# Gate logits of a routed result from VectorE instead of TensorE, with GpSimd's index copies moved ahead

## The chip, the core and the metric

The program runs on one core of a Trainium2 chip. The metric is the device time of one execution in microseconds (us). Five engines run side by side: TensorE (PE in the profile, its weight loads PEld), VectorE (DVE), ScalarE (ACT), GpSimd (POOL) and SyncE (SP), which issues transfers. Engines wait for each other on semaphores. Transfers run on 16 DMA engines. PSUM is the memory that TensorE writes to, in banks of 512 fp32 numbers per partition; SBUF is the working memory.

## What is computed

A chunked attention gives 2304 rows of 512 numbers. Then come two mixtures of 8 experts. Each row goes to the expert with its largest gate logit, through two products with a ReLU between, and comes back scaled by a gate:

```
logits = x @ w_gate                       # 512 -> 8
e_idx = argmax(logits); gate_w = softmax(logits)[e_idx]
h = maximum(x[mask] @ w1[e], 0)           # 512 -> 1024
ye = h @ w2[e]                            # 1024 -> 512
out[mask] = gate_w * eom * ye             # mixture 1, eom a sigmoid of a second gate
out[i] = gate_w[i] * y[expert, pos]       # mixture 2, with a capacity of 576 rows per expert
```

The second mixture needs `logits = x @ moe2_w_gate` of the first mixture's result before it can route.

## The kernel before

In the attention (18 blocks of 128 rows) the first mixture's logits are made too, and the first 16 pieces of expert weights are loaded. Then both mixtures (m = 0 and 1) sort their rows by expert into tiles of 128, 20 tiles in each here, and go through them one a step.

Products are in fp32 precision by parts: each operand is split into a rounded high part and a low remainder, and three matmuls (high by high, low by high, high by low) make one product (`product`, L988 to L990). An expert's weights are 8 pieces of 128x1024: SyncE loads a piece into a ring of 4, ScalarE rounds it (`wh`), GpSimd subtracts (`wl`, L427). Two experts are held at a time. A piece of expert e may overwrite expert e-2 once the last tile of that one is through.

Step g on each engine, in program order:

- TensorE: transposes of the hidden rows of tile g (L1010); the first product of tile g+1 (24 matmuls), in which, in mixture 1, the four transposes of result g-1 (L1029) and its logit matmuls (L1035) are set; the transposes of the gathered rows of tile g+2 (L983); the second product of tile g (24 matmuls), into one PSUM bank.
- VectorE: splits the hidden rows into high and low (L809, L815), in mixture 1 copies the transposed result (L823) and its 8 logits (L834), ReLU of tile g+1 (L792), splits the gathered rows of tile g+2 (L800, L802), scales result g into `y` (L830) once the scatter of result g-1 has landed.
- GpSimd: loads three bounds that say how many pieces are due (`due`, L435 to L440); makes the low parts of up to 4 pieces (`split`); scatters result g-1 (`scatter`: index copy L526, transfer L532); gathers the rows of tile g+3 (`gather`: index copy L515, transfer L518), which needs TensorE's row transposes of tile g+2 done; makes the low parts of up to 4 more pieces.

A table computed from the routing sets the pieces of each step, so an expert's weights are ready about when its first tile is. `y`, the gathered rows `xg` and both index columns (`sidx`, `gidx`) have one buffer each. The queue of every engine is in order: what waits holds all that is behind it.

Of the kernel before, what the change touches and what calls it, by code (L numbers as in the profile page):

```python
# [6 lines left out]
BF16 = mybir.dt.bfloat16  # L7
# [6 lines left out]
P = 128  # L14
# [9 lines left out]
def build(nc, q, k, v, wg1, wog1, w1a, w2a, wg2, w1b, w2b, cap, out):  # L24
# [29 lines left out]
    with ctx:  # L54
# [32 lines left out]
        wgate2 = sb("wgate2", [P, DC, E])  # L87
# [57 lines left out]
        at_pos = sb("at_pos", [P, 2, P, NH2], BF16)  # L145
        in_tile = sb("in_tile", [P, 2, NTAB, NH2], BF16)
        at_tile = sb("at_tile", [P, 2, NV, NTAB, NH2], BF16)
        at_gate = sb("at_gate", [P, 2, NG, NTAB, NH2], BF16)
        xg = sb("xg", [P, ROW])
        yT = sb("yT", [P, DC, P])  # L150
        h = sb("h", [P, F])
# [12 lines left out]
        hTh = sb("hTh", [P, FC, P], F32R)  # L164
        hTl = sb("hTl", [P, FC, P], F32R)
# [13 lines left out]
        ps_h, ps_hT, ps_y, ps_yT, ps_xT = b01, b23, b45[:, 0:BANK], b45[:, BANK:2 * BANK], b6  # L179
# [5 lines left out]
        s_w = sem("s_w")  # L185
        s_zero = sem("s_zero")
# [60 lines left out]
        yT_done = sem("yT_done")  # L247
        yT_here = sem("yT_here")
        yl_done = sem("yl_done")
        yl_here = sem("yl_here")  # L250
# [6 lines left out]
        def at(x, g):  # L257

            return x[:, g:g + 1] if isinstance(g, int) else x[:, bass.ds(g, 1)]

# [44 lines left out]
        def _(sp):  # L305
# [3 lines left out]
            sp.dma_start(wgate2[:, :, :], wg2.rearrange("(c p) e -> p c e", p=P)).then_inc(s_w, 16)  # L309
# [89 lines left out]
        def _(pool):  # L399
# [56 lines left out]
            for m in range(2):  # L456
# [79 lines left out]
                def step(g, ahead=True):  # L536
# [8 lines left out]
                    split(middle, hi)  # L545

                step(0)
                with pool.Fori(1, total - 2) as g:
                    step(g)
                step(total - 2, ahead=False)  # L550
                step(total - 1, ahead=False)
                scatter(total - 1)
# [5 lines left out]
        def _(act):  # L558
# [49 lines left out]

            exponentials(0)
# [16 lines left out]
        def _(dve):  # L626
            dve.wait_ge(s_const, 2)
            dve.wait_ge(s_w, 64)
# [60 lines left out]
            for m in range(2):  # L689
# [92 lines left out]
                def gates_copy():  # L782
                    dve.wait_ge(gates_done, m + 1)
                    link(nc.vector.tensor_reduce(gates[m][:, :], ps_gate[:, 0:NG * NTAB].rearrange("p (a c) -> p c a", a=NG),
                                                 AX.X, ALU.add))

# [32 lines left out]
                def y_copy(j):  # L819
                    dve.wait_ge(yT_done, j + 1)  # L820
                    if reached(j, 1):
                        dve.wait_ge(yl_done, j)
                    nc.vector.tensor_copy(yT[:, :, :], ps_yT.rearrange("p (c t) -> p c t", c=DC)).then_inc(yT_here, 1)  # L823

                def scaled(j):
# [4 lines left out]
                    nc.vector.tensor_scalar(y[:, 0:D], ps_y, at(gates[m], j), None, ALU.mult).then_inc(y_here[m], 1)  # L830

                def logits_copy(j):
                    dve.wait_ge(yl_done, j + 1)
                    nc.vector.tensor_copy(y[:, D:ROW], ps_yT[:, 0:E]).then_inc(yl_here, 1)  # L834

                def step(g, head=False, tail=False):
                    if head:
                        dve.wait_ge(routed, m + 1)
                        x_split(0)
# [8 lines left out]
                    if m == 0 and reached(g, 1):  # L848
                        y_copy(g - 1)
# [3 lines left out]
                    if m == 0 and reached(g, 1):  # L853
                        logits_copy(g - 1)
# [11 lines left out]
        def _(pe):  # L866
            pe.wait_ge(s_const, 2)
            pe.wait_ge(s_w, 64)
# [71 lines left out]
            for m in range(2):  # L940
# [72 lines left out]
                def second_product(g, first, before):  # L1013
                    pe.wait_ge(wl_here, before + PX)
                    if reached(g, 1):
                        pe.wait_ge(y_here[m], g)
                    for half in range(2):
                        pe.wait_ge((hT0_here, hT1_here)[half][m], g + 1)
                        for c in range(half * FC // 2, (half + 1) * FC // 2):
                            last = product(ps_y, hTh[:, c, :], hTl[:, c, :], (first, D * F // P // BANK + c),  # L1020
                                           start=(c == 0), stop=(c == FC - 1))
                    last.then_inc(y_done[m], 1)

                def result_T(j):
                    pe.wait_ge(y_here[m], j + 1)
                    if reached(j, 1):
                        pe.wait_ge(yl_here, j)
                    for c in range(DC):
                        last = nc.tensor.transpose(ps_yT[:, c * P:(c + 1) * P], y[:, c * P:(c + 1) * P], ident[:, :])  # L1029
                    last.then_inc(yT_done, 1)  # L1030

                def result_logits(j):
                    pe.wait_ge(yT_here, j + 1)
                    for c in range(DC):
# [57 lines left out]
```

## Time and profile before

| | |
|---|---|
| median of 3 runs | 767.88 us (763.83, 767.88, 769.28) |
| profiled execution | 763.25 us, span 761.4 us, mean granted TensorE clock 0.934 of full |
| busy share of the span | PE 86%, PEld 71%, POOL 55%, DVE 45%, ACT 22% |
| first mixture | steps from 145 us, last scatter 436.83 us |
| second mixture | steps from 480 us, last scatter 751.99 us |
| chain that ended last | PE 63%, POOL 10%, issue 9%, DVE 6%, DMA 5% |

The span is the time from the first to the last instruction. A busy share is an average over stages: attention up to 117 us, routing to 134 us, first mixture to 440 us, routing to 468 us, second mixture to the end.

### The profile page before, as it was taken

The page shows a single profiled execution, that of the slowest core. Times are in us where ns is not written, and L with a number is a line of the kernel's source. Part 1 is how long each engine was busy: PE and PEld are TensorE (multiplying, and loading weights), DVE is VectorE, ACT ScalarE, POOL GpSimd, SP SyncE. Part 2 cuts the span into 40 slices and gives each one's busy share as a digit, 9 for nine tenths or more (in the row PEclk, how much of TensorE's full clock was granted, in tenths as well). Part 3 has the DMA queues.
Part 4 walks back from the last instruction along what each step waited for, and adds up shares of the span by engine and source line. Part 5 has one row for each costly group of instructions (what it writes and reads, how often), then busy time and mean ns, then how long its engine had stood idle before and what let it go on. Part 6 is the DMA issues. An engine that isn't in the chain of part 4 may idle for free.

```text
span 761.4 us, 15861 instructions
## 1 busy us (share of the span) xinstructions
PE 654.5 (86%) x4742; PEld 540.3 (71%) x4743; DVE 344.6 (45%) x634; ACT 170.2 (22%) x205; POOL 420.5 (55%) x351
## 2 busy tenths in 40 slices
PE   4799984899999999998998623999999999999553
PEld 3698973688887888887876422788888878887442
DVE  2465657345444545434433266454545354532240
ACT  1465650002230222213224200002122210233300
POOL 1355553113786638778877524116648763679760
PEclk9999996799999999999999755999999999999796
DMA  7999988011454324454455314014225533355510
GB/s 168 277 277 269 291 261 280 28 34 60 154 207 167 110 78 165 169 191 155 170 189 173 125 15 135 29 42 151 96 92 182 167 131 111 95 183 187 190 42 22
DMA packets 79694, 111.71 MB, mean 147 GB/s; under 512 B 28249, under 2 KB 46681, under 8 KB 79664
## 3 DMA queue, kind: packets, MB, share of 16 engines
q1 hardware_dynamic: 69344, 86.05, 36.7%
q0 software_dynamic: 8000, 25.17, 9.9%
q8 instruction: 21, 0.34, 0.2%
q10 hardware_dynamic: 2320, 0.07, 0.2%
q14 instruction: 9, 0.07, 0.0%
HBM read 92.48 MB, written 20.00 MB: 148 GB/s over the span
## 4 chain that ended last, share of the span: by engine, by line
PE 63%; POOL 10%; issue 9%; DVE 6%; DMA 5%; POOLq 4%; ACT 1%; SPq 0%; ACTq 0%; DVEq 0%
PE b L988 15%; PE b L989 14%; PE b L990 14%; POOL wl L427 8%; PE b L915 5%; PE b L1010 3%; PE b L937 2%; DMA qin<-in_q 2%; PE b L983 2%; PE b L1035 2%; PE b L929 2%; PE b L892 1%; PE b L884 1%; DVE owner L761 1%; POOLq L427 1%
## 5 line engine op out<-in xcount | busy, mean ns | idle before, releaser
L427 POOL TENSOR_TENSOR wl<-ring,wh (+1 forms) x128 | 302.4, 2390 | 41.1 <-ACT wh L600 21.0
L600 ACT CAST wh<-ring 128x1024 f32 (+1 forms) x112 | 112.8, 1047 | 482.4 <-PE b L990 389.8
L988 PE MATMUL b<-wh,xTh 128*128 x320 | 134.8, 421 | 5.9 <-DVE xTl L802 3.7
L988 PE MATMUL b<-wh,hTh 128*128 x320 | 132.0, 413 | 7.5 <-DVE hTl L815 7.5
L830 DVE TENSOR_SCALAR y<-b,gates 128x512 f32<-128x512 f32 x40 | 30.0, 750 | 227.1 <-PE b L990 102.5
L989 PE MATMUL b<-wh,xTl 128*128 x320 | 128.7, 402 | 0.0
L989 PE MATMUL b<-wh,hTl 128*128 x320 | 128.6, 402 | 0.0
L990 PE MATMUL b<-wl,hTh 128*128 x320 | 127.5, 398 | 0.0
L990 PE MATMUL b<-wl,xTh 128*128 x320 | 127.5, 398 | 0.0
L792 DVE TENSOR_SCALAR h<-b 128x512 f32<-128x512 f32 x80 | 54.8, 689 | 77.9 <-PE b L990 77.7
L988 PEld LDWEIGHTS b<-wh,hTh 128*128 128x128 f32 x320 | 61.5, 192 | 21.1 <-issue 7.7
L988 PEld LDWEIGHTS b<-wh,xTh 128*128 128x128 f32 x320 | 61.3, 192 | 19.2 <-issue 7.4
L990 PEld LDWEIGHTS b<-wl,hTh 128*128 128x128 f32 x320 | 61.2, 191 | 15.0
L990 PEld LDWEIGHTS b<-wl,xTh 128*128 128x128 f32 x320 | 61.2, 191 | 14.8
L989 PEld LDWEIGHTS b<-wh,hTl 128*128 128x128 f32 x320 | 61.5, 192 | 12.7
L989 PEld LDWEIGHTS b<-wh,xTl 128*128 128x128 f32 x320 | 61.5, 192 | 11.2
L518 POOL DMA_INDIRECT xg<-x,gidx x36 | 37.9, 1052 | 31.6 <-POOL gidx L515 31.6
L815 DVE TENSOR_TENSOR hTl<-b,hTh 128x512 fp32r<-128x512 f32 x80 | 52.6, 679 | 0.0
L809 DVE CAST hTh<-b 128x512 fp32r<-128x512 f32 x80 | 51.1, 680 | 0.0
L983 PE MATMUL b<-ident,xg 128*128 128x128 f32 x168 | 26.8, 284 | 25.4 <-DMA xg<-x,gidx 12.3
L532 POOL DMA_INDIRECT x<-y,sidx x20 | 20.5, 1024 | 49.8 <-DVE y L834 26.6
L431 POOL DMA_DIRECT2D x<-xrow x18 | 10.3, 570 | 64.5 <-DVE xrow L664 64.5
(142 smaller groups left out, 667.4 us busy)
## 6 DMA issues: line engine op xcount, KB each, us to landing
ring<-in_moe_w SPq DMA_DIRECT2D x128, 512.0 KB, 3.3
vin<-in_v SPq DMA_DIRECT2D x72, 64.0 KB, 4.7
x<-xrow POOLq DMA_DIRECT2D x18, 256.0 KB, 5.9
out<-zeros SPq DMA_DIRECT2D x18, 256.0 KB, 3.2
qin<-in_q SPq DMA_DIRECT2D x6, 512.0 KB, 7.3
kin<-in_k SPq DMA_DIRECT2D x6, 512.0 KB, 7.5
qin<-in_q SPq DMA_DIRECT2D x2, 384.0 KB, 8.2
kin<-in_k SPq DMA_DIRECT2D x2, 384.0 KB, 8.3
```

The source lines that it names most:

```text
L427: nc.gpsimd.tensor_tensor(low, src, high.bitcast(F32), ALU.subtract).then_inc(wl_here, 1)
L518: nc.gpsimd.indirect_dma_start(xg[:, 0:src.shape[1]], None, src, bass.IndirectOffsetOnAxis(ap=gidx[:, 0:1], axis=0), bounds_check=N - 1, o ...
L600: nc.scalar.copy(dst, ring[:, i % RING]).then_inc(wh_here, 1)
L792: nc.vector.tensor_scalar_max(h[:, cols], ps_h[:, cols], 0.0).then_inc((h0_here, h1_here)[half][m], 1)
L809: nc.vector.tensor_copy(hTh[:, chunks, :], ps_hT[:, half * BANK:(half + 1) * BANK].rearrange("p (c t) -> p c t", t=P)).then_inc((hTh0_here ...
L815: nc.vector.tensor_tensor(hTl[:, chunks, :], ps_hT[:, half * BANK:(half + 1) * BANK].rearrange("p (c t) -> p c t", t=P), hTh[:, chunks, :] ...
L830: nc.vector.tensor_scalar(y[:, 0:D], ps_y, at(gates[m], j), None, ALU.mult).then_inc(y_here[m], 1)
L915: last = nc.tensor.matmul(b01[e * DH:(e + 1) * DH, u * BANK + g * P:u * BANK + (g + 1) * P], src[:, n // 2 % QS, g, e, u, :], ident[:, :], ...
L983: last = nc.tensor.transpose(ps_xT[:, c * P:(c + 1) * P], xg[:, c * P:(c + 1) * P], ident[:, :])
L988: nc.tensor.matmul(dst, high, weights(wh, *wt), start=start, stop=False)
L989: nc.tensor.matmul(dst, low, weights(wh, *wt), start=False, stop=False)
L990: return nc.tensor.matmul(dst, high, weights(wl, *wt), start=False, stop=stop)
```

## The change

Four edits go together.

1. The second mixture's logits no longer come from TensorE. The gate matrix is handed over transposed (8 rows of 512) and broadcast to all partitions in one transfer from ScalarE's queue (`wg2_rows`, 2 MB in SBUF). VectorE makes logit e of a result as one instruction: PSUM result times gate times row e, and the sum over 512 numbers (`scalar_tensor_tensor` with `accum_out`), eight per tile. The transposes, the copy of the transposed result and the logit matmuls go.
2. The second product alternates between two PSUM banks (`result_bank`), in both mixtures. In mixture 1 result g-1 is scaled at the end of VectorE's step g, behind the eight sums; `y_here` starts at one more, so the second product of tile g waits for the scaling of g-2.
3. In mixture 1 the scatter is two steps behind (`behind`).
4. GpSimd copies the index columns at the end of a step, for the next step's gather and scatter (`next_gather`, `next_scatter`), instead of right before each transfer.

Some SBUF tiles are laid over others to make room.

```diff
+        def result_bank(eng, j):
+            if isinstance(j, int):
+                return b45[:, j % 2 * BANK:(j % 2 + 1) * BANK]
+            return b45[:, bass.ds(eng.snap((j % 2) * BANK), BANK)]
...
+                def next_gather(g):
+                    if reached(g, 4):
+                        pool.wait_ge(g_in[m], g * 16)
+                    nc.gpsimd.tensor_copy(gidx[:, :], at(gather_at[m], g)).then_inc(gi_here[m], 1)
+
+                def next_scatter(g):
+                    if reached(g, 1):
+                        pool.wait_ge(y_out[m], g * 16)
+                    nc.gpsimd.tensor_copy(sidx[:, :], at(scatter_at[m], g)).then_inc(si_here[m], 1)
                 def gather(g):
-                    if reached(g, 1):
-                        pool.wait_ge(g_in[m], g * 16)
-                        pool.wait_ge(xT_done[m], g)
-                    nc.gpsimd.tensor_copy(gidx[:, :], at(gather_at[m], g)).then_inc(gi_here[m], 1)
+                    pool.wait_ge(xT_done[m], g)
...
                 def scatter(g):
-                    if reached(g, 1):
-                        pool.wait_ge(y_out[m], g * 16)
-                    nc.gpsimd.tensor_copy(sidx[:, :], at(scatter_at[m], g)).then_inc(si_here[m], 1)
                     pool.wait_ge(si_here[m], g + 1)
-                    pool.wait_ge(y_here[m], g + 1)
-                    if m == 0:
-                        pool.wait_ge(yl_here, g + 1)
+                    pool.wait_ge(y_here[m], g + 2)
...
                     lo, middle, hi = due(m, g)
                     split(lo, middle)
-                    if reached(g, 1):
-                        scatter(g - 1)
+                    if reached(g, behind):
+                        scatter(g - behind)
                     if ahead:
                         gather(g + 3)
                     split(middle, hi)
+                    if ahead:
+                        next_gather(g + 4)
+                    if reached(g, behind - 1):
+                        next_scatter(g + 1 - behind)
+                behind = (2, 1)[m]
...
+            act.wait_ge(lg_done, NT)
+            act.wait_ge(o_done, NT)
+            act.wait_ge(x_here, NT)
+            act.dma_start(wg2_rows[:, :, :].rearrange("p e d -> p (e d)"),
+                          wg2.rearrange("e d -> (e d)").unsqueeze(0).partition_broadcast(P)).then_inc(wg2_in, 16)
...
+                def next_logits(j, experts):
+                    dve.wait_ge(y_done[m], j + 1)
+                    dve.wait_ge(y_here[m], j + 1)
+                    for e in experts:
+                        if e >= 2:
+                            dve.wait_ge(next_lg_here, j * E + e - 1)
+                        nc.vector.scalar_tensor_tensor(
+                            out=(unread, b7)[e % 2][:, :], in0=result_bank(dve, j), scalar=at(gates[m], j), in1=wg2_rows[:, e, :],
+                            op0=ALU.mult, op1=ALU.mult, accum_out=next_lg[:, e:e + 1]).then_inc(next_lg_here, 1)
...
                     if m == 0 and reached(g, 1):
-                        logits_copy(g - 1)
+                        next_logits(g - 1, range(0, E // 2))
                     if not tail:
                         relu(g + 1, 1)
                         x_split(g + 2)
-                    scaled(g)
+                    if m == 0 and reached(g, 1):
+                        next_logits(g - 1, range(E // 2, E))
+                        scaled(g - 1)
                     if m == 0 and tail:
-                        y_copy(g)
-                        logits_copy(g)
+                        next_logits(g, range(E))
+                    if m == 1 or tail:
+                        scaled(g)
```

GpSimd's queue in the loop of the first mixture, from the first group of pieces to the next step's bounds, before (`sidx` and `gidx` are the index columns, `y_out0` and `g_in0` count landed scatters and gathers):

```order
L526 ISA [waits y_out0]
L526 COPY sidx<-scatter_at 128x1
L532 DMA x<-y,sidx 2304x520 [waits yl_here,si_here0,y_here0]
L513 ISA
L515 ISA [waits xT_done0,g_in0]
L515 COPY gidx<-gather_at 128x1
L518 DMA xg<-x,gidx 128x512 [waits gi_here0]
```

The same place now; the rows left out are the second group of pieces:

```order
L544 DMA x<-y,sidx 2304x520 [waits si_here0,y_here0]
L532 REGISTER_ALU
L535 DMA xg<-x,gidx 128x512 [waits xT_done0,gi_here0]
...
L522 ISA [waits g_in0]
L522 COPY gidx<-gather_at 128x1
L527 REGISTER_ALU
L528 ISA [waits y_out0]
L528 COPY sidx<-scatter_at 128x1
```

The copies and the waits for landed transfers have moved from in front of the transfers to the end of the step, ahead of the next step's bounds.

VectorE's queue in the same loop, second half of a step, before (`h`, `xTh`, `xTl` belong to later tiles, `y` is the scaled result):

```order
L792 TENSOR_SCALAR h<-b 128x512 [waits hT0_done0,h0_done0]
L834 COPY y<-b 128x8 [waits yl_done]
L792 TENSOR_SCALAR h<-b 128x512 [waits hT1_done0,h1_done0]
L797 REGISTER_ALU
L800 CAST xTh<-b 128x512 [waits h1_done0,xT_done0]
L802 TENSOR_TENSOR xTl<-b,xTh 128x512 [waits xTh_here0]
L829 REGISTER_ALU [waits y_done0]
L830 ISA [waits y_out0]
L830 TENSOR_SCALAR y<-b,gates 128x512
```

And the end of that step now, behind the split of the gathered rows (four sums stand ahead of the second ReLU in the same way):

```order
L832 TENSOR_TENSOR xTl<-b,xTh 128x512 [waits xTh_here0]
L866 REGISTER_ALU [waits y_here0,y_done0]
L867 SCALAR_TENSOR_TENSOR unread,next_lg<-b,gates,wg_rows 128x512 [waits next_lg_here]
L866 REGISTER_ALU
L867 SCALAR_TENSOR_TENSOR b,next_lg<-b,gates,wg_rows 128x512 [waits next_lg_here]
...
L853 REGISTER_ALU [waits y_done0]
L855 REGISTER_ALU [waits y_out0]
L856 COPY y<-next_lg 128x8 [waits next_lg_here]
```

The wait for the scatter's landing still ends VectorE's step, now behind four more 128x512 instructions and for the result of one step earlier.

## Rows read from the trace of the kernel before

**Rows 1.** Timeline of TensorE, steps of both mixtures: start us, us, engine, instruction.
```profile
173.10 1.03 PE L1010 MATMUL b<-ident,h 128*128 128x128 f32 x8
...
180.91 0.60 PE L983 MATMUL b<-ident,xg 128*128 128x128 f32 x4
...
186.94 1.03 PE L1010 MATMUL b<-ident,h 128*128 128x128 f32 x8
...
581.38 1.03 PE L1010 MATMUL b<-ident,h 128*128 128x128 f32 x8
593.89 1.03 PE L1010 MATMUL b<-ident,h 128*128 128x128 f32 x8
```

**Rows 2.** Timeline of GpSimd, one full step; in brackets idle time before, and its releaser.
```profile
284.07 9.43 POOL L427 TENSOR_TENSOR wl<-ring,wh  x4 [1.57 <-issue]
...
294.54 1.03 POOL L532 DMA_INDIRECT x<-y,sidx  x1 [0.92 <-PE b L983]
...
296.63 1.06 POOL L518 DMA_INDIRECT xg<-x,gidx  x1 [0.86 <-POOL gidx L515]
299.30 9.43 POOL L427 TENSOR_TENSOR wl<-ring,wh  x4 [1.62 <-issue]
```

**Rows 3.** Timeline of GpSimd, first mixture, steps 2 to 4 and step 9.
```profile
182.82 1.05 POOL L518 DMA_INDIRECT xg<-x,gidx  x1 [0.85 <-POOL gidx L515]
185.49 9.45 POOL L427 TENSOR_TENSOR wl<-ring,wh  x4 [1.61 <-ACT wh L600]
...
202.59 9.47 POOL L427 TENSOR_TENSOR wl<-ring,wh  x4 [3.43 <-ACT wh L600]
...
279.35 1.03 POOL L532 DMA_INDIRECT x<-y,sidx  x1 [7.77 <-DVE y L834]
```

**Rows 4.** The page's costliest groups, two of VectorE: busy, mean ns, idle before.
```profile
L830 DVE TENSOR_SCALAR y<-b,gates 128x512 f32<-128x512 f32 x40 | 30.0, 750 | 227.1 <-PE b L990 102.5
...
L815 DVE TENSOR_TENSOR hTl<-b,hTh 128x512 fp32r<-128x512 f32 x80 | 52.6, 679 | 0.0
```

**Rows 5.** Windows: length, PE, PEld, DVE, ACT, POOL busy, clock, DMA share, GB/s.
```profile
115.00:120.00 5.00, 2.02 (x15) 1.59 (x14) 2.35 (x8) 0.91 (x2) 1.09 (x2) 0.81 0.99 369
...
130.00:135.00 5.00, 3.30 (x20) 2.61 (x18) 2.70 (x16) 0.00 (x0) 1.11 (x1) 0.50 0.19 52
...
186.00:200.00 14.00, 14.00 (x74) 11.66 (x73) 6.66 (x11) 0.00 (x0) 11.36 (x8) 1.00 0.51 171
```

**Rows 6.** All 36 gathers of line L518: issue to landing.
```profile
DMA to landing us min/median/max: 3.2/3.4/4.2
```

**Rows 7.** Timeline of GpSimd, end of the first mixture.
```profile
404.99 9.47 POOL L427 TENSOR_TENSOR wl<-ring,wh  x4 [1.61 <-ACT wh L600]
...
415.50 1.03 POOL L532 DMA_INDIRECT x<-y,sidx  x1 [0.92 <-POOL sidx L526]
...
428.56 1.02 POOL L532 DMA_INDIRECT x<-y,sidx  x1 [0.94 <-POOL sidx L526]
431.84 0.18 POOL L526 COPY sidx<-scatter_at 128x1 int32 x1 [2.25 <-DMA x<-y,sidx]
436.83 0.98 POOL L532 DMA_INDIRECT x<-y,sidx  x1 [4.82 <-DVE y L834]
```

**Rows 8.** Timeline of VectorE, the scaling that waits for that scatter.
```profile
419.36 0.75 DVE L830 TENSOR_SCALAR y<-b,gates 128x512 f32<-128x512 f32 x1 [7.17 <-DMA x<-y,sidx]
```

**Rows 9.** Timeline of GpSimd, second mixture.
```profile
563.65 0.18 POOL L515 COPY gidx<-gather_at 128x1 int32 x1 [3.70 <-PE b L983]
...
567.51 9.47 POOL L427 TENSOR_TENSOR wl<-ring,wh  x4 [1.72 <-ACT wh L600]
...
611.34 1.06 POOL L518 DMA_INDIRECT xg<-x,gidx  x1 [0.89 <-POOL gidx L515]
...
653.20 0.18 POOL L515 COPY gidx<-gather_at 128x1 int32 x1 [4.21 <-PE b L983]
...
736.98 1.03 POOL L532 DMA_INDIRECT out<-y,sidx  x1 [0.94 <-POOL sidx L526]
```

More of the change, by code:

```diff
@@ L144, in build, with routed_by @@
             xrow = early("xrow", [P, XS, G, 2, DH])
[L145 to L148, printed above, removed]
+        with ExitStack() as routing:
+            def routed_by(name, shape):
+                return routing.enter_context(nc.sbuf_tensor(name, shape, BF16))
+            at_pos = routed_by("at_pos", [P, 2, P, NH2])
+            in_tile = routed_by("in_tile", [P, 2, NTAB, NH2])
+            at_tile = routed_by("at_tile", [P, 2, NV, NTAB, NH2])
+            at_gate = routed_by("at_gate", [P, 2, NG, NTAB, NH2])
+        hTh = sb("hTh", [P, FC, P], F32R)
+        hTl = sb("hTl", [P, FC, P], F32R)
+        h = sb("h", [P, F])
         xg = sb("xg", [P, ROW])
-        yT = sb("yT", [P, DC, P])
-        h = sb("h", [P, F])
+        wg2_rows = sb("wg2_rows", [P, E, D])
+        unread = sb("unread", [P, D])
+        next_lg = sb("next_lg", [P, E])
         y = sb("y", [P, ROW])
@@ L185, in build @@
         s_w = sem("s_w")
+        wg2_in = sem("wg2_in")
+        next_lg_here = sem("next_lg_here")
         s_zero = sem("s_zero")
@@ L545, in step @@
                     split(middle, hi)
+                    if ahead:
[3 more added lines that the diff above has]
+                behind = (2, 1)[m]
+                next_gather(3)
                 step(0)
-                with pool.Fori(1, total - 2) as g:
+                if m == 0:
+                    step(1)
+                    step(2)
+                with pool.Fori((3, 1)[m], total - 2) as g:
                     step(g)
@@ L551, in _ @@
                 step(total - 1, ahead=False)
+                if m == 0:
+                    scatter(total - 2)
+                    next_scatter(total - 1)
                 scatter(total - 1)
@@ L785, in gates_copy @@
                                                  AX.X, ALU.add))
+                    dve.sem_inc(y_here[m], 1)
                 def relu(j, half):
@@ L838, in step @@
                         dve.wait_ge(routed, m + 1)
+                        if m == 0:
+                            dve.wait_ge(wg2_in, 16)
                         x_split(0)
@@ L867, in _ @@
             pe.wait_ge(s_const, 2)
-            pe.wait_ge(s_w, 64)
+            pe.wait_ge(s_w, 48)
             pe.wait_ge(s_vones, 1)
@@ L1019, in second_product @@
                         for c in range(half * FC // 2, (half + 1) * FC // 2):
-                            last = product(ps_y, hTh[:, c, :], hTl[:, c, :], (first, D * F // P // BANK + c),
+                            last = product(dst, hTh[:, c, :], hTl[:, c, :], (first, D * F // P // BANK + c),
                                            start=(c == 0), stop=(c == FC - 1))
                     last.then_inc(y_done[m], 1)
[L1024 to L1034, printed above, removed]
-                        last = nc.tensor.matmul(ps_yT[:, 0:E], yT[:, c, :], wgate2[:, c, :],
-                                                start=(c == 0), stop=(c == DC - 1))
-                    last.then_inc(yl_done, 1)
                 def step(g, head=False, tail=False):
@@ L1053, in step @@
                     if not tail:
-                        first_product(g + 1, 0, *following, chunks=range(0, DC // 2))
-                    if m == 0 and reached(g, 1):
-                        result_T(g - 1)
-                    if not tail:
-                        first_product(g + 1, 0, *following, chunks=range(DC // 2, DC))
-                        first_product(g + 1, 1, *following, chunks=range(0, DC // 2))
-                    if m == 0 and reached(g, 1):
-                        result_logits(g - 1)
-                    if not tail:
-                        first_product(g + 1, 1, *following, chunks=range(DC // 2, DC))
+                        first_product(g + 1, 0, *following)
+                        first_product(g + 1, 1, *following)
                         rows_T(g + 2)
                     second_product(g, *this)
-                    if m == 0 and tail:
-                        result_T(g)
-                        result_logits(g)
                 expert_steps(pe, m, step)
```

31 lines of the change are left out of this document (9 added, 22 removed).

## The prediction, made before the changed kernel ran

> **What bounds the kernel now.** I read, in this order, the page's busy shares, the order of TensorE's work in one step, and then GpSimd's timeline, because GpSimd both makes the low parts of the weights and issues every gather and scatter. TensorE is busy 86% of the span, which looks like the bound. Its step in the first mixture takes 13.84 us (173.10 to 186.94), in the second 12.51 us, where no logits are made [rows 1]. The difference, 1.33 us, is what the transposes and the logit matmuls of a result cost on TensorE.
>
> GpSimd tells another story. While it splits weights it is nearly full: from one group of four pieces to the next it takes 15.23 us (284.07 to 299.30): 9.43 for the pieces, 1.04 from their end to the scatter (index copy and the wait for it), 1.03 for the scatter, 1.06 to the gather, 2.67 from the gather's start to the next piece, in which it loads the next step's bounds [rows 2]. That is more than either step of TensorE. In the first mixture the program has 15 such groups in 20 steps. Steps 4 and 14 hold two groups, steps 5, 7, 9 and 15 none, so GpSimd catches up there, and it waits only now and then: 3.43 us for weights at step 4, 7.77 us for a result at step 9 [rows 3]. From about 299 us it waits for nobody, and TensorE's steps stretch. So GpSimd has little to spare in the first mixture even at TensorE's slow pace.
>
> **What the change does, part by part.**
>
> TensorE loses 1.33 us in each of 19 steps of the first mixture. By itself that would be -25 us. It is worth that only if everything beside it keeps a 12.51 us step.
>
> VectorE loses one 128x512 copy and gains eight multiply-and-sums per result. The nearest rows are the pointer-scaled read of a PSUM bank, 750 ns, and the subtraction of PSUM and SBUF, 679 ns [rows 4]. Two such in a row start about 0.6 to 0.7 us apart. I take 0.68; bounds are 0.60 and, should the sum cost a second pass over 512 elements, 1.25. VectorE was busy 6.66 us in a 14 us stretch [rows 5]. Without the copy (0.68) and with 8 x 0.68 it comes to 11.4 us, under 12.51, so in mid-loop it is hidden; the bound at which it decides is (12.51 - 6.0)/8 = 0.81. The Trainium skill, in VectorE: DVE Perf Modes, section Two Vector instructions with no wait between them, says that an operation that writes out its accumulator is two instructions. No row here shows what the second one costs; one that added 0.1 us would put VectorE at the edge, at 12.2.
>
> GpSimd's index copies no longer stand between pieces and scatter, nor between scatter and gather: -1.04 and -1.06 us (0.1 stays for dispatch). But the copy for gather g+4 now waits for the landing of gather g+3, which has been issued just before it, and it stands ahead of the next step's loads. The gathers landed 3.4 us after their start in the middle, 3.2 to 4.2 [rows 6]. Before, the same wait came one step later, when the data had long landed. So from a gather's start to the next piece it is 2.67 + 3.4 = 6.07 us; the 0.2 us by which the loads started after the gather pays for the copies. A full step becomes 9.43 + 1.03 + 0.1 + 6.07 = 16.63 us, **1.4 us more than now**. Where a second group follows the gather (steps 4 and 14) the landing is hidden: 9.43 + 0.1 + 1.03 + 1.05 + 9.43 + 0.3 = 21.3. A step without pieces costs 7.2.
>
> A rule against the trace here: the Trainium skill (DMA: Bandwidth & Descriptors, Anatomy of one DMA) fits such a DMA as 2.0 us plus bytes over 436e3 per us. For 128 rows of 2 KB that is 2.6 us, not the 3.4 of the rows, and with 0.8 us less per full step the sum below would come out near zero. The rows are of the same gathers, so they decide.
>
> The two result banks and the scatter two steps behind free TensorE from the last scaling, and let GpSimd scatter without its waits for a result. They give slack, not throughput: GpSimd's queue is longer than its covering work.
>
> **First mixture.** The gather of step 2 waits for the row transposes, which ended at 181.51 (180.91 + 0.60) [rows 1]. Two steps before that are 1.33 shorter: 178.85, so the gather starts at 178.95 and the first piece of step 3 at 185.0 (before: 185.49 [rows 3]). Steps 3 to 17: nine full ones 149.7, two double ones 42.6, four empty ones 28.8. Step 18's pieces start at 406.1; they did at 404.99 [rows 7]. The whole gain of TensorE is gone by then: 16 steps of 12.51 from 171.8 would have it at step 18 at 372, so it waits.
> The end of the mixture: pieces to 415.6, scatter; the next index copy waits for its landing, 3.28 us as in 428.56 to 431.84 [rows 7], then copy and loads 2.6 (2.67 in [rows 2]), pieces 9.43: scatter 17 starts at 430.9. The scaling of tile 18 starts 3.86 later (415.50 to 419.36 was the same wait [rows 8]) and takes 0.75. Only behind it stand the eight sums of tile 19, 5.4 us, and its copy and scaling, 0.85. Scatter 19 goes out at 441.9 instead of 436.83: **+5.1 us**.
>
> **Second mixture.** TensorE's work is the same. Step 6's index copy was released by the transposes at 563.65; now the gather is, and the next piece comes 6.07 later, 569.8 instead of 567.51. Two full steps (7 and 8) and the 10.6 us to the gather in step 9 bring gather 12 to 613.6 instead of 611.34, and TensorE waits for that one: +2.3 for all behind. The gather released at 653.20 now starts at 655.5, pieces of step 14 at 661.6, step 15, a double one, at 678.2, step 16 at 699.5, step 17 at 716.1, step 18 at 732.8, and the scatter behind them at 742.3 instead of 736.98 [rows 9]. What follows that scatter is as before: **+5.3 us**.
>
> **Costed at nothing.** The 2 MB broadcast of the gate weights goes out at about 117 us, when the DMA engines are at 0.99 and is wanted at 135, when they were at 0.19 [rows 5]; at 369 GB/s it is 5.7 us of their time, and the bound is 0 to +4 if it lands late or holds up the writes of x1. One small load less in front of the first Q load: 0 to -0.5. Prefetched copies, bank choice by register: hidden in waits.
>
> Sum: +10.4 us. The profiled run took 763.25 us, 4.6 below the median of 767.88; the change is added to the median: **778 us** (for a run like the profiled one, 773.5).
>
> **Rivals.**
> 1. **The landing wait costs little** (faster). If GpSimd does not stand still for the landing, a full step is 9.43 + 1.03 + 0.1 + 2.67 = 13.2 us, near TensorE's 12.5. Nine such steps, two double ones of 21.3 and four empty ones of 3.8 are 177 us, under 15 of TensorE's 12.51 (188), so TensorE's pace holds: of the 25 us some 18 stay behind the tail's +5, and in the second mixture the chain of gathers and pieces at its end gives some 2 more: 748 us. For it: the copies' 2.1 us per step are really removed. Against it: the queue is in order, the wait names the gather just issued, and at the end of the first mixture the trace shows GpSimd standing 2.25 us for a landing [rows 7]. It decides where the landing adds less than 1.4 us to a step. 12%.
> 2. **A break-even.** With 0.5 us less than 16.6 in a full step, by a faster landing or shorter loads, the 13 affected steps of the first mixture and 6 of the second give back 6 to 10 us: 768 to 772. 18%.
> 3. **VectorE becomes the bound.** At 1.25 us per sum its step is 6.0 + 10.0 = 16 us against GpSimd's mean of 14.7 over steps 3 to 17: 1.3 x 18 more, and 4.6 in the tail: about 805 us. Of sums from two fp32 SBUF operands the Trainium skill (Vector Engine (DVE) Microarchitecture Reference, Points that are easy to get wrong) says that they run at half rate; here one operand is in PSUM, so it speaks only weakly for this. 8%.
> 4. **The forecast**, GpSimd longer by 1.0 to 1.9 us in a full step, +4 to +18: 62%.
>
> **Numbers.** A measurement of this kernel can tell about 1% from no change. Faster by over 1% is rival 1: 0.12. Within 1% are rival 2 and the lower quarter of the forecast (up to +7.7 us): 0.33. Slower is the rest: 0.55. The range leaves out rivals 1 and 3: 766 to 789.
>
> **What will show it.** In the profile after: GpSimd's groups of four pieces 16.6 us apart where now 15.2; an index copy ahead of each gather with a wait for that gather's landing of about 2.3 us; the sums 0.65 to 0.75 us apart; TensorE at 12.5 us a step up to about step 6 and then waiting, for weights or rows; the last scatter of the first mixture near 442. If the groups are 13 to 14 us apart I am wrong about the wait; if the sums are over 0.8 apart, about VectorE.

## The result, and the profile after

The changed kernel took **821.05 us** (median of four runs, 817.24 to 823.19) against 765.86 us for the kernel before on the same chip: ratio 1.0716, 95% interval 1.0645 to 1.0787. I had forecast 778 us, in a range of 766 to 789. Of all executions in this document one stands out, 1320.85 us in number 3 below, and the ratios leave it out. The direction and its place were right, the size was not: GpSimd's queue became the bound, but by far more per step than I had worked out.

| | before | forecast | after |
|---|---|---|---|
| gather of step 2, first mixture | 182.82 | 178.95 | 185.76 |
| first piece of step 3 | 185.49 | 185.0 | 191.93 |
| pieces of step 18 | 404.99 | 406.1 | 436.36 |
| last scatter, first mixture | 436.83 | 441.9 | 474.92 |
| last scatter, second mixture | 751.99 | 762.4 | 811.63 |

TensorE is no longer nearly full. The page after, its busy shares and its chain of work that ended last:

```profile
PE 650.5 (79%) x4502; PEld 532.4 (65%) x4503; DVE 451.3 (55%) x934; ACT 171.3 (21%) x205; POOL 419.7 (51%) x353
...
PE 39%; issue 15%; DMA 15%; POOL 13%; DVE 7%; POOLq 7%; SPq 2%; ACT 1%; DVEq 0%; ACTq 0%
```

The chain held 63% PE before, 9% "issue" (an engine that waits for nothing the profile shows), 5% DMA and 4% POOLq (GpSimd's sequencer). It now holds 15%, 15% and 7% of the last three. Of the DMA share 7% are the gathers alone (the page's chain by line), so much of this is GpSimd's queue and what it waits for, while GpSimd itself is busy only 51%. So read its timeline, not its share. A full step after, where [rows 2] had 15.23 us from group to group (start us, us, engine, line, operation; in brackets the idle time before and what ended it):

```profile
314.03 9.46 POOL L435 TENSOR_TENSOR wl<-ring,wh  x4 [2.74 <-issue]
323.64 1.02 POOL L544 DMA_INDIRECT x<-y,sidx  x1
324.96 1.03 POOL L535 DMA_INDIRECT xg<-x,gidx  x1 [0.30 <-issue]
328.91 0.18 POOL L522 COPY gidx<-gather_at 128x1 int32 x1 [2.91 <-DMA xg<-x,gidx]
329.09 0.18 POOL L528 COPY sidx<-scatter_at 128x1 int32 x1
332.03 9.46 POOL L435 TENSOR_TENSOR wl<-ring,wh  x4 [2.75 <-issue]
```

From 314.03 to 332.03 is 18.00 us: 9.46 for the pieces, 0.15, 1.02 for the scatter, 0.30, then 3.95 from the gather's start to the index copy that waited for its landing, 0.36 for two copies, 2.75 for the loads of the next bounds. None of these stands beside another. The waits that grew (engine, line, waited for: total us, times, longest):

```profile
ACT wh L624 <- DMA ring<-in_moe_w: 160.2, 60, 17.7
DVE y L857 <- DMA out<-y,sidx: 114.6, 11, 16.3
POOL gidx L522 <- DMA xg<-x,gidx: 95.0, 33, 3.9
DVE y L856 <- DMA x<-y,sidx: 71.0, 13, 7.8
...
PE b L1026 <- DVE hTl L845: 47.6, 13, 10.5
```

The third row is the landing wait, 2.9 us on average in 33 of the 38 index copies. The second and fourth are VectorE waiting for the landing of scatters, which GpSimd issues late, and the first is ScalarE waiting for weights. The last is TensorE waiting for the split of `h` behind that wait of VectorE, and in two steps behind something I had not foreseen (numbers 4 to 7).

TensorE did at first what the forecast said. The transposes of gathered rows and of `h`, timeline of TensorE:

```profile
171.88 0.60 PE L1021 MATMUL b<-ident,xg 128*128 128x128 f32 x4
...
184.27 0.60 PE L1021 MATMUL b<-ident,xg 128*128 128x128 f32 x4
...
318.30 1.04 PE L1048 MATMUL b<-ident,h 128*128 128x128 f32 x8
328.80 0.97 PE L1021 MATMUL b<-ident,xg 128*128 128x128 f32 x4 [4.00 <-DMA xg<-x,gidx]
...
338.97 1.04 PE L1048 MATMUL b<-ident,h 128*128 128x128 f32 x8
```

Its early step is 12.4 us (171.88 to 184.27), 1.4 less than in [rows 1]; later it waits, 20.7 us from 318.30 to 338.97. Apart from a stop near 230 us it kept 12.4 us until 304.55, longer than the "about step 6" of the forecast.

VectorE does the sums at the price forecast:

```profile
234.79 0.73 DVE L867 SCALAR_TENSOR_TENSOR unread<-b,gates,wg_rows 128x512 f32<-128x512 f32 x1
235.46 0.07 DVE L867 DVE_READ_ACCUMULATOR unread<-b,gates,wg_rows 128x1 f32 x1
235.46 0.75 DVE L867 SCALAR_TENSOR_TENSOR b<-b,gates,wg_rows 128x512 f32<-128x512 f32 x1
```

They start 0.67 us apart. The second instruction that the Trainium skill (VectorE: DVE Perf Modes, Two Vector instructions with no wait between them) announces is there as DVE_READ_ACCUMULATOR, but it lies wholly beside the next sum and shows no cost of its own: the scaling (L857), which has no accumulator, also starts 0.66 us before what follows it (231.14 to 231.80).

### The profile page after: what moved, and what is told of

The parts are those of the page before. It is cut to its first block, busy times and chain, and to the rows that moved or that the text cites. A ratio compares the mean times of both kernels' runs of the same rounds, so it can differ in the third digit from the quotient of the medians.

```text
span 821.1 us, 15856 instructions
## 1 busy us (share of the span) xinstructions
PE 650.5 (79%) x4502; PEld 532.4 (65%) x4503; DVE 451.3 (55%) x934; ACT 171.3 (21%) x205; POOL 419.7 (51%) x353
## 4 chain that ended last, share of the span: by engine, by line
PE 39%; issue 15%; DMA 15%; POOL 13%; DVE 7%; POOLq 7%; SPq 2%; ACT 1%; DVEq 0%; ACTq 0%
POOL wl L435 11%; PE b L1026 9%; PE b L1027 8%; PE b L1028 8%; DMA xg<-x,gidx 7%; PE b L953 4%; DMA x<-y,sidx 2%; PE b L975 2%; DMA ring<-in_moe_w 2%; PE b L1048 2%; POOLq L435 2%; PE b L967 1%; PE b L1021 1%; PE b L930 1%; DMA qin<-in_q 1%
## 5 line engine op out<-in xcount | busy, mean ns | idle before, releaser
L1026 PE MATMUL b<-wh,hTh 128*128 x320 | 140.6, 440 | 48.6 <-DVE hTl L845 47.6
L1027 PE MATMUL b<-wh,hTl 128*128 x320 | 135.9, 425 | 0.0
L1028 PE MATMUL b<-wl,hTh 128*128 x320 | 135.0, 422 | 0.0
L857 DVE TENSOR_SCALAR y<-b,gates 128x512 f32 (+1 forms) x40 | 29.9, 747 | 158.0 <-DMA out<-y,sidx 114.6
L1028 PEld LDWEIGHTS b<-wl,hTh 128*128 128x128 f32 x320 | 66.1, 207 | 16.8
L1027 PEld LDWEIGHTS b<-wh,hTl 128*128 128x128 f32 x320 | 66.5, 208 | 14.7
L867 DVE SCALAR_TENSOR_TENSOR b<-b,gates,wg_rows 128x512 f32<-128x512 f32 x80 | 60.2, 753 | 0.0
L867 DVE SCALAR_TENSOR_TENSOR unread<-b,gates,wg_rows 128x512 f32<-128x512 f32 x80 | 59.4, 743 | 0.3 <-DVE y L857 0.3
L856 DVE COPY y<-next_lg 128x8 f32<-128x8 f32 x20 | 18.4, 919 | 71.2 <-DMA x<-y,sidx 71.0
L1021 PEld LDWEIGHTS b<-ident,xg 128*128 128x128 f32 x168 | 21.7, 151 | 52.9 <-DMA xg<-x,gidx 33.7
```

The source lines that it names most:

```text
L856: nc.vector.tensor_copy(y[:, D:ROW], next_lg[:, :])
L857: nc.vector.tensor_scalar(y[:, 0:D], result_bank(dve, j), at(gates[m], j), None, ALU.mult).then_inc(y_here[m], 1)
L867: nc.vector.scalar_tensor_tensor(out=(unread, b7)[e % 2][:, :], in0=result_bank(dve, j), scalar=at(gates[m], j), in1=wg2_rows[:, e, :], op ...
L1021: last = nc.tensor.transpose(ps_xT[:, c * P:(c + 1) * P], xg[:, c * P:(c + 1) * P], ident[:, :])
L1026: nc.tensor.matmul(dst, high, weights(wh, *wt), start=start, stop=False)
L1027: nc.tensor.matmul(dst, low, weights(wh, *wt), start=False, stop=False)
```

## The experiments

Theory A: the wait for the gather's landing, in a row with the loads of the bounds on GpSimd's queue, makes the whole loss. Rival B: the sums on VectorE, with the later scaling and scatter, make it. The kernel before took 766.34 to 767.63 us (medians) in these measurements; ratios are to its runs on the same chip. Numbers 1 to 4 ran on one chip, 5 to 8 on a second, 9 to 12 on a third. Differences of times between these groups, and to the 821.05 us, are across chips, and good to a few us only.

**1. The index copies back in front of their transfers**, all else as changed.

```diff
                 def gather(g):
+                    next_gather(g)
...
                 def scatter(g):
+                    next_scatter(g)
...
-                    if ahead:
-                        next_gather(g + 4)
-                    if reached(g, behind - 1):
-                        next_scatter(g + 1 - behind)
```

> The changed kernel, with the index copies right in front of their transfers again, as before; sums, two banks and the scatter two steps behind stay. Theory A (the copies' wait for the landing, ahead of the bounds' loads, costs the time): a full step of GpSimd is back at 15.2 to 15.4 us and an empty one under 6, so steps 3 to 17 of the first mixture take about 207 us instead of 244 and the second mixture is back at 315 instead of 337: 758 to 768 us, at or a little below the kernel before (ratio 0.99 to 1.00). Theory B (the sums on VectorE, or their place ahead of the scaling, cost most of it): over 800 us, ratio 1.04 or more.

Measured: 765.06 us, ratio 0.9986 (0.9948 to 1.0023). A full step of GpSimd is back at 15.57 us:

```profile
310.05 9.47 POOL L435 TENSOR_TENSOR wl<-ring,wh  x4 [1.82 <-ACT wh L619]
...
321.64 0.20 POOL L522 COPY gidx<-gather_at 128x1 int32 x1
322.70 1.06 POOL L536 DMA_INDIRECT xg<-x,gidx  x1 [0.87 <-issue]
325.62 9.42 POOL L435 TENSOR_TENSOR wl<-ring,wh  x4 [1.85 <-issue]
```

The copy for the gather (0.20) no longer waits for anything: the gather it asks for was issued a step earlier. Sums, banks and the later scatter together cost nothing here, and gain nothing either, as GpSimd's step is back where it was. (Two held copies, found in number 4, are part of this time; number 6 is the same kernel without them.)

**2. Only the copies moved, in the kernel before**: the logits stay on TensorE.

```diff
...
+                    if ahead:
+                        next_gather(g + 4)
+                    next_scatter(g)
...
```

> The kernel before, with only the index copies moved to the end of the step. Theory A: full steps of 18 us and empty ones of 9, as in the changed kernel: both mixtures as slow as there, 800 to 815 us (ratio 1.05 to 1.065). Theory B: within 1.5% of the kernel before.

Measured: 821.8 us, ratio 1.0718 (1.0635 to 1.08), the whole loss of the change without any of its sums, and over the 800 to 815 expected. Its full step, 17.96 us:

```profile
314.28 9.44 POOL L427 TENSOR_TENSOR wl<-ring,wh  x4 [2.50 <-issue]
...
325.21 1.03 POOL L527 DMA_INDIRECT xg<-x,gidx  x1 [0.31 <-issue]
329.36 0.18 POOL L514 COPY gidx<-gather_at 128x1 int32 x1 [3.11 <-DMA xg<-x,gidx]
...
332.24 9.43 POOL L427 TENSOR_TENSOR wl<-ring,wh  x4 [2.52 <-issue]
```

The two runs settle A against B: one part alone gives all of the time, the rest without it none.

**3 and 8. The copies in the middle of a group of pieces, kernel before.** A copy ahead is cheap where pieces stand between the gather and the wait for its landing. The same kernel was measured twice.

```diff
-                    split(lo, middle)
+                    cut = pool.snap((lo + middle) // 2)
+                    split(lo, cut)
+                    if ahead:
+                        next_gather(g + 3)
+                    if reached(g, 1):
+                        next_scatter(g - 1)
+                    split(cut, middle)
```

> The kernel before, with both index copies placed between the second and third piece of a group, so that the wait for the landed gather and the copies' own latency are both covered by pieces. Theory A: a full step of GpSimd is 13.5 to 14.2 us, under TensorE's 13.84 in the first mixture: that mixture is TensorE-bound and gains 8 to 10 us, the second 3 to 6: 750 to 757 us (ratio 0.98 to 0.99). Theory B says nothing of it: within 1%.

> The kernel before with the index copies among the pieces, once more for a profile at full clock: 753 us; full steps of GpSimd 13.5 to 14.2 us where they run back to back, TensorE's steps of the first mixture at 13.84 us throughout.

Measured: 753.53 us, ratio 0.981 (0.9744 to 0.9877), and again 751.39 us, 0.9774 (0.9702 to 0.9847). The first is the median of five executions: 1320.85 us, and four of 747.34 to 754.5. In the profile of number 8 most of TensorE's steps in the first mixture take 13.84 or 13.85 us, a few 14.6 to 15.1: there TensorE is the bound.

**4. The same in the changed kernel.**

```diff
+                    if reached(g, behind):
+                        next_scatter(g - behind)
+                    split(cut, middle)
```

> The changed kernel with the index copies among the pieces in the same way. Theory A: a full step of GpSimd is 13.5 to 14.2 us, TensorE's 12.51; steps 3 to 17 of the first mixture take 190 to 200 us instead of 244: 735 to 748 us (ratio 0.96 to 0.975). Theory B: over 790 us.

Measured: 759.7 us, 0.9892 (0.9827 to 0.9958). This fell short: with the logits off TensorE it should have beaten number 3, and is slower. The trace names what held it. VectorE:

```profile
215.65 7.43 DVE L857 COPY y<-next_lg 128x8 f32<-128x8 f32 x1 [4.13 <-DMA x<-y,sidx]
222.99 0.74 DVE L858 TENSOR_SCALAR y<-b,gates 128x512 f32 x1
...
246.69 0.17 DVE L857 COPY y<-next_lg 128x8 f32<-128x8 f32 x1
```

GpSimd beside it:

```profile
213.69 9.34 POOL L435 TENSOR_TENSOR wl<-ring,wh  x4
```

TensorE:

```profile
218.07 0.39 PE L1029 MATMUL b<-wl,xTh 128*128 x1
226.00 0.79 PE L1027 MATMUL b<-wh,hTh 128*128 x1 [7.10 <-DVE hTl L846]
226.59 0.63 PE L1028 MATMUL b<-wh,hTl 128*128 x1
```

Windows of the same kernel (from:to, length, busy time of PE, PEld, DVE, ACT and POOL, granted clock, DMA share, GB/s):

```profile
205.00:215.00 10.00, 10.00 (x51) 8.25 (x50) 6.48 (x17) 3.19 (x4) 9.50 (x8) 1.00 0.73 238
215.00:225.00 10.00, 3.89 (x20) 3.02 (x18) 9.36 (x5) 3.68 (x4) 8.68 (x7) 0.96 0.63 197
225.00:232.00 7.00, 6.00 (x16) 4.78 (x17) 6.97 (x17) 1.52 (x2) 5.34 (x4) 0.57 0.38 130
```

A copy of eight numbers that takes 0.17 us where no piece runs beside it stands for 7.43, until GpSimd's four pieces, made without a gap, end at 223.03. The split of `h` queues behind it, TensorE stands 7.10 us. Behind that idle time its granted clock falls from 1.00 (2.4 GHz) to a mean of 0.57 over 7 us, so most of them at the lower level of 1.2 GHz, with matmuls of 0.63 us instead of 0.39. Of the 20 copies in the profile four stood 6.05 to 7.70 us, 28.3 us in sum.

**5, 6 and 7. The eight numbers written by an instruction that reads PSUM too**, in the changed kernel, in number 1 and in number 4.

```diff
-                        nc.vector.tensor_copy(y[:, D:ROW], next_lg[:, :])
+                        nc.vector.scalar_tensor_tensor(
+                            out=y[:, D:ROW], in0=result_bank(dve, j)[:, 0:E], scalar=0.0, in1=next_lg[:, :],
+                            op0=ALU.mult, op1=ALU.add)
```

> The changed kernel, with VectorE's copy of the 8 sums into the result row written as PSUM times zero plus the sums, so that it is no copy from SBUF to SBUF. Theory A1 (that copy is held while GpSimd makes pieces back to back, 7.49 and 6.45 us in the two double steps, but GpSimd's queue is the bound of this kernel): no instance over 0.3 us, time 3 to 8 us less, 813 to 818 us. Theory C (the held copy is what costs the changed kernel its time): 20 us or more less.

> The changed kernel with the index copies back in front of their transfers, and the copy of the sums from PSUM. Theory A1: the two held copies of 9.12 and 9.22 us go, and what waits for them on TensorE; a full step of GpSimd stays 15.5 us, so of 18 us some 5 to 12 show: 753 to 760 us. Theory C: 745 us or less.

> The changed kernel with the index copies among the pieces, and the copy of the sums from PSUM. Here TensorE bounds most of the first mixture and the held copies (7.43, 7.70, 7.08, 6.05 us) stand in its way: 22 to 30 us less than with the held copies, 730 to 740 us (ratio to the kernel before 0.955 to 0.965). If the held copies are covered by other waits: 750 to 760 us.

Measured: 818.74 us (1.0633, 1.0561 to 1.0704), 759.59 us (0.9872, 0.9805 to 0.9939) and **729.6 us (0.9487, 0.9426 to 0.9548)**. Number 5 is just above the 813 to 818 expected, number 7 just below its 730 to 740. In number 7 all twenty take the same time (line, count, ns min/median/max):

```profile
L857 DVE SCALAR_TENSOR_TENSOR y<-b,next_lg x20: 166/167/168, 171.0 to 407.6; 128x8 f32<-128x8 f32 x20
```

The hold costs little where GpSimd is the bound (2.3 us from the changed kernel to number 5, whose intervals overlap, 5.5 from number 1 to number 6, whose intervals do not quite) and 30 us where TensorE is (number 4 to number 7). GpSimd's full step in number 7, 12.39 us from 270.79 to 283.18 (its groups are now two and two):

```profile
270.79 4.75 POOL L435 TENSOR_TENSOR wl<-ring,wh  x2 [1.74 <-issue]
275.49 0.18 POOL L522 COPY gidx<-gather_at 128x1 int32 x1
...
282.00 1.03 POOL L535 DMA_INDIRECT xg<-x,gidx  x1 [0.31 <-issue]
283.18 4.76 POOL L435 TENSOR_TENSOR wl<-ring,wh  x2 [0.16 <-issue]
```

Against number 8, measured beside it, which has the same order of copies and the logits on TensorE, the sums on VectorE, with the two banks and the later scatter, are worth 751.39 - 729.6 = 21.8 us: nearly the 25 us of TensorE's 19 x 1.33. Most of TensorE's steps in the first mixture are now 12.38 or 12.39 us, for 13.84 or 13.85 there.

**9. A quarter of the weights' bytes.** Why did gathers land after 4.0 to 4.4 us behind pieces, and not after 3.4?

```diff
+                        dst, w = dst[:, :, 0:D // 4], w[:, :, 0:D // 4]
+                    else:
+                        dst, w = dst[:, 0:PIECE // 4], w[:, 0:PIECE // 4]
```

> The changed kernel, but in both mixtures SyncE loads only a quarter of each piece of weights (128 rows of 1 KB instead of 4 KB); what lies in the rest of the buffers is multiplied as it is, so the output is not the reference's, and only the first mixture, whose routing does not hang on them, is read. Open is why a gather took 4.0 to 4.4 us to land behind a group of pieces and 3.4 in a step without. Theory: the weights' loads share the DMA engines with it; with a quarter of their bytes it lands after about 3.4 us, its index copy waits about 2.3 instead of 2.9 us, and a full step of GpSimd takes 17.3 to 17.5 us instead of 18.1. Rival: it is the scatter issued just ahead of it; then it stays at 4.0 to 4.4 and 18.1. If the landing falls below 3.2, part of the 3.4 was the weights' too.

Measured (one run, 786.1 us; first mixture read): full step 17.61 us (304.78 to 322.39).

```profile
315.73 1.03 POOL L538 DMA_INDIRECT xg<-x,gidx  x1 [0.31 <-issue]
319.28 0.18 POOL L525 COPY gidx<-gather_at 128x1 int32 x1 [2.52 <-DMA xg<-x,gidx]
```

From the gather's start to the copy 3.55 us, in the next step 3.49, against 3.95 in the changed kernel; of this the landing is 3.4 us against 3.8. The step is 0.1 us over the figure expected.

So the scatter just ahead does not do it alone. Nor do the weights' bytes alone: with all of them the gathers behind a group landed after 3.2 to 3.6 us in the first mixture of the kernel before, but for one of 4.0, and after 3.2 to 3.5 in number 1, but for two of 3.9. What the early copies change is the time of the gather. It starts 1.47 us behind the end of the pieces (323.49 to 324.96) and no longer 3.13 (293.50 to 296.63), and then flies while the DMA engines are busy. Windows of the changed kernel, of the kernel before and of number 9 from a gather's start on (columns as in number 4):

```profile
325.00:328.80 3.80, 0.00 (x0) 0.00 (x0) 0.75 (x3) 1.59 (x2) 0.99 (x1) 1.00 0.76 262
296.60:300.10 3.50, 3.50 (x20) 2.91 (x19) 0.31 (x1) 1.19 (x2) 1.85 (x2) 1.00 0.40 136
315.70:319.20 3.50, 0.03 (x1) 0.03 (x1) 1.72 (x4) 1.04 (x1) 1.03 (x1) 1.00 0.51 176
```

The engines' share is 0.76 in the first and 0.40 in the second. Twice, behind the second group of a double step, the gather of the changed kernel started 2.9 us behind the pieces (at 234.11 and 392.54), 1.3 us behind the scatter as ever, and landed after 3.3 us. So the nearness to the pieces, and to the loads that they set free, goes with the longer landing; a run that changes this alone was not made.

**10. The copies behind the loads of the bounds.** The landing then runs beside the loads.

```diff
                     lo, middle, hi = due(m, g)
+                    if ahead:
+                        next_gather(g + 3)
+                    if reached(g, behind):
+                        next_scatter(g - behind)
```

> The changed kernel with the two index copies behind the loads of the step's bounds, ahead of its first group of pieces (same gathers, scatters, banks and sums). The landing wait (2.9 us) then runs beside the 2.75 us of loads. Theory (it is the wait in a row with the loads that costs, not the copies or their number): full step 9.46 + 0.15 + 1.03 + 0.31 + about 4.2 + 0.36 = 15.5 to 15.8 us, 2.4 less than in the changed kernel, about that of the kernel before; time 765 to 778 us. Rival (the gather or the copies themselves take the time, wherever they stand): about 821 us.

Measured: 771.19 us, 1.0073 (1.0042 to 1.0104). The full step, 15.53 us from 301.35 to 316.88:

```profile
301.35 9.47 POOL L435 TENSOR_TENSOR wl<-ring,wh  x4 [0.37 <-issue]
...
312.29 1.03 POOL L535 DMA_INDIRECT xg<-x,gidx  x1 [0.30 <-issue]
316.13 0.18 POOL L522 COPY gidx<-gather_at 128x1 int32 x1 [2.81 <-DMA xg<-x,gidx]
...
316.88 9.43 POOL L435 TENSOR_TENSOR wl<-ring,wh  x4 [0.37 <-issue]
```

The same copies, the same wait, in another place of the row: 50 us less than the changed kernel's 821.05. That is the sharpest form of theory A.

**11. Twelve sums per result in number 7**, four of them made twice.

```diff
-                            op0=ALU.mult, op1=ALU.mult, accum_out=next_lg[:, e:e + 1]).then_inc(next_lg_here, 1)
+                            op0=ALU.mult, op1=ALU.mult,
+                            accum_out=(twice if i % 3 == 2 else next_lg)[:, e:e + 1]).then_inc(next_lg_here, 1)
```

> The kernel with the copies among the pieces and the copy from PSUM (729.6 us), but with twelve sums per result instead of eight (four are made twice, into an unused tile). It asks where VectorE decides. Theory: its step is 6.0 + 12 x 0.67 = 14.0 us, over TensorE's 12.5, and its chain of logits at the end of the first mixture is 2.7 us longer: up to 17 x 1.5 + 2.7 = 28 us more, less what GpSimd already holds up; 745 to 758 us. Rival (VectorE has slack enough, as GpSimd or TensorE bounds each step): at most the 2.7 us of the tail more, 730 to 733.

Measured: 754.35 us, 0.9882 (0.9844 to 0.9921), 24.8 us over number 7 and 24.2 over number 12, which ran beside it. The step of VectorE, from one first split of `h` to the next, is 13.87 us:

```profile
271.44 1.28 DVE L841 CAST hTh<-b 128x512 fp32r<-128x512 f32 x2
...
285.31 1.28 DVE L841 CAST hTh<-b 128x512 fp32r<-128x512 f32 x2
```

With twelve sums VectorE is the bound, with eight it is not.

**12. The wait for the gate weights at the first sum** instead of at the head of the mixture, in number 7.

```diff
+                        if m == 0:
+                            dve.wait_ge(wg2_in, 16)
```

> The kernel with the copies among the pieces and the copy from PSUM (729.6 us), with VectorE's wait for the 2 MB of gate weights moved from the head of the first mixture to the first sum. In the changed kernel the second gather started at 142.91 us against 136.13 before, and part of that is this wait. Theory: -1 to -3 us, 727 to 729. Rival (the start is late for the DMA traffic itself, not for the wait): 729.6 as before.

Measured: 730.2 us, 0.9559 (0.9526 to 0.9592): no gain. The gather that stands at 160.99 us in the changed kernel stood at 154.4 to 160.1 in the profiles of seven other kernels with the same head (numbers 1, 4 to 7, 10 and 11), and at 155.0 to 156.5 in three without the gate weights' transfer. The changed kernel's very first gather was already 4.8 us late (134.75 for 129.97), where the seven had 127.3 to 134.6: that part is the run's. The rest goes with the landing of this first gather, 6.1 us; it was 3.7 to 6.2 in the seven, 3.4 and 3.5 without the transfer, but 3.4 in number 12 too. Whether that is the transfer's is not shown.

## Why the prediction was wrong in size

**TensorE, -1.33 us a step: right.** 12.4 us a step while rows came in time; then it waited, as forecast, though later.

**VectorE, 0.68 us a sum: right.** 0.67, and number 11 shows the edge where it was put: 6.0 + 12 x 0.67 = 14.0 us against 13.87 measured. Rival 3 fell.

**GpSimd, a full step of 16.63 us: this step failed.** The seven full steps of the first mixture that stand alone took 127.71 us, 18.24 on average. The working counted 3.4 us of landing and 2.67 from gather to pieces, 6.07 in sum. Where no pieces stood ahead, at step 2, it was 6.17 (185.76 to 191.93). In the loop it was 7.07 (324.96 to 332.03):

- From the gather's start to the index copy it took 3.95 us, not 3.4: 3.8 of landing (3.7 to 4.8 right behind a group of the first mixture) and 0.15 until the copy began. The 3.4 was a fair reading of the kernel before, also behind a group. But the change itself brought the gather to within 1.5 us of the pieces, into the traffic of the weights' loads (number 9).
- The two index copies take 0.36 us. I had let the 0.2 us between gather and loads pay for them; nothing paid.
- The loads took 2.75 us, near the 2.67 that I had from [rows 2].
- Two gaps of 0.15 and 0.30 us stand where I had 0.1 for dispatch.

That is 0.55 + 0.36 + 0.08 + 0.35 = 1.34 of the 1.37 us between 16.63 and the 18.00 shown. The rest of the average comes in with the other steps (two of the last took 18.56 and 18.67).

**Double and empty steps.** An empty step behind a full one took 9.04 us from gather to gather (280.28 to 289.32), not 7.2, for the same reasons. The two pairs of a double and an empty step took 30.74 and 30.77, not 28.5; the two pairs of a full and an empty one 28.69 and 26.52, not 23.8. Over steps 3 to 17 of the first mixture: 7 x 1.61 + 2 x 2.26 + (55.21 - 47.66) = 11.3 + 4.5 + 7.5 = 23.3 us more than the 221.1 forecast (244.43 measured). I had taken the empty steps for slack; such a pair at 26.5 to 28.7 is longer than two of TensorE's 12.5, so they gave none back.

**The sum of the miss.** At the last scatter of the first mixture 33.0 us: 6.9 at the start, 23.3 in steps 3 to 17, 2.8 in the tail, where the copy behind a scatter began 4.69 us after the scatter's start, for 3.28 in [rows 7]:

```profile
445.89 1.04 POOL L544 DMA_INDIRECT x<-y,sidx  x1 [0.15 <-issue]
450.58 0.18 POOL L528 COPY sidx<-scatter_at 128x1 int32 x1 [3.65 <-DMA x<-y,sidx]
...
474.92 0.98 POOL L544 DMA_INDIRECT x<-y,sidx  x1 [3.61 <-DVE y L857]
```

The second mixture took 21.5 us more than before instead of 5.3. I had let TensorE take the lead again at [rows 9] 563.65 and 653.20, where GpSimd waited for transposes. With pairs of a full and an empty step at 26.2 to 27.1 us it was not early enough for that, and from 557.58 to 699.25 it waited for no transposes at all. The miss is thus 33.0 + 16.2 = 49.2 us at 811.63, against 762.4.

**Start, 0 to +4.** The profiled run had +6 at the gather of 160.99. By the other profiles 4.8 of it was the run's; for the rest the cause is open (number 12).

**Costed at nothing.** The prefetched copies were named as hidden in waits; they were not. The copy of the eight numbers had a price I did not look for, since before it read PSUM. In the changed kernel it stood long twice (7.49 and 6.45 us) and hid behind GpSimd, as number 5 shows.

**The rivals.** None came true for the changed kernel: its landing wait cost more than forecast, not less. The time of rival 2, 768 to 772 us, is what number 10 takes, but by another order of the queue and with a step of 15.5 us. What rival 1 hoped for, 748 us, comes once the landing is off the queue: 759.7 in number 4 and 729.6 in number 7.

**The rule weighed there.** The fit of the Trainium skill (DMA: Bandwidth & Descriptors, Anatomy of one DMA) gave 2.6 us for a gather, as an estimate. No landing here agrees: 3.4 us with a quarter of the weights' bytes, 3.8 with all of them. The rows were nearer than the rule, and still too low for the new place.

## What to carry to other kernels

A prefetch on an in-order queue moves its wait as well: the copy for the next gather stood behind the gather whose landing it needed, so a wait that had been met long ago became 2.9 us in nearly every step. Put it where at least the landing time of independent work lies between (here two pieces, 4.7 us, or the bounds' loads), and price every item of the queue in a row. A duration read from the trace before holds for the order before: here the new order put the gather where the DMA engines were busier, and it landed 0.4 us later. And when a VectorE copy no longer reads PSUM but SBUF, ask what GpSimd is doing beside VectorE: the copy of eight numbers, from SBUF to SBUF where the one before had read PSUM, cost 30 us once the queue was mended.

## What the runs showed of the hardware

**A small fp32 copy from SBUF to SBUF on VectorE can stand for a whole run of GpSimd's instructions.** Beside 7.43 us above, in number 1 it stood 9.22 us:

```profile
354.83 9.22 DVE L851 COPY y<-next_lg 128x8 f32<-128x8 f32 x1 [4.38 <-DMA x<-y,sidx]
```

```profile
354.77 9.24 POOL L435 TENSOR_TENSOR wl<-ring,wh  x4
```

It began 0.06 us after the four pieces and ended with them. The Trainium skill (SBUF — State Buffer, Who interferes with whom) says that a copy on VectorE can enter a mode in which it and GpSimd exclude each other, and that whoever issues first has the shared ports for the whole instruction while the other blocks. The trace agrees on the exclusion, but the copy waited for four instructions of 2.37 us in a row, not for one. It does not always: in the changed kernel one that met a group at 242.25 us stood 0.83 us, until the first piece ended. The profiles of the changed kernel and of numbers 1 and 4 hold eight copies that stood over 6 us. Each met a run of pieces (with the index copies in it) that began within 0.03 us of the end of the transfer instruction ahead of it. The ones that stood 0.2 to 2.1 us met a run with a gap of 0.1 us or more before it, mostly over 1.2. Why that should decide is open. The form with one operand in PSUM never stood (168 ns at most in number 7), as the same section has it for an instruction with at most one input in SBUF outside those modes.

**A landing is not one number.** The same gather of 128 rows landed after 3.4 us with a quarter of the weights' bytes, after 3.8 with all of them 1.5 us behind the pieces, and after 3.5 with all of them 3.1 us behind (296.63 in the kernel before). A scatter in the tail landed after 4.5.
